# Attention in half-batch units of one pair of heads, and a first MLP that waits for half of batch 0

## The chip, the cores and the metric

The kernel runs on one core of a Trainium2 chip. The metric is the device time of one execution in microseconds (us), lower is better. TensorE (PE) multiplies and writes PSUM banks; VectorE (DVE), ScalarE (ACT) and GpSimd (POOL) work on what it leaves; the SP queue issues DMAs. Every engine runs its instructions in program order and waits on semaphores, so an instruction that waits also holds all that stand behind it on its engine.

## The reference, cut to what matters

Three stages follow each other. `q`, `k`, `v` are 4 batches x 8 heads x 576 positions x 64.

```python
q_d, k_d, v_d = means over groups of 4 positions      # 144 rows
out_up    = repeat(softmax_attention(q_d, k_d, v_d), 4)
out_local = softmax_attention(q, k, v, mask=|i - j| < 4)
x = (out_up + out_local) -> 2304 tokens x 512
h = x @ w_in;  g = s * relu(h)**2 + b;  y = g @ w_out           # d_ff 2048
out = ((y @ w_a) * (y @ w_b)) @ w2                              # d_ff 1536
```

Both MLPs are computed in float32 precision from pairs of a high and a low part ("hi" and "lo"), three matmuls for each product.

## The kernel before, in words

**Attention** goes by pairs of heads over a whole batch: 16 pairs (n), each 576 positions wide. A pair goes through three softmaxes, called jobs: POOLED (144 x 144, both halves together), LOCAL0 (windows 0 to 2 of 96 queries, 102 keys each) and LOCAL1 (windows 3 to 5). The steps of a job: PE turns q and k (`turn`, L467), ACT copies them out (L701, L703), DVE sums groups of four (L868), PE makes scores (L478, L493), DVE adds the mask and takes maxima (L875, L888, L890), POOL subtracts (L1073), ACT takes exponentials (L713, L719), DVE sums and inverts (L896 to L900), POOL normalises (L1081), PE turns the weights (L512, L517), ACT copies them (L726), PE multiplies with v (L538, L546), DVE adds pooled and local (L907, L917), and the result is split into hi on ACT (L776) and lo on DVE (L976).

**Boot.** The four pairs of batch 0 run alone, through 30 ticks, pair p six ticks behind pair p-1, in two sets of buffers ("kits") used in turn. In between, six of the sixteen weight blocks of the first MLP are split (hi on ACT L771, lo on DVE L971 or POOL L1088). The first `up_matmuls` stands at tick 28.

**First MLP.** 8 chunks of 288 tokens, 16 blocks each: 128 slots. In slot s PE does `attention(n, 2s)`, `up_matmuls(s)` (12 matmuls, L617, into the one bank HB), `attention(n, 2s+1)`, `down_matmuls(s-2)` (12 matmuls, L632). So an odd tick lies behind the up matmuls of its slot and an even tick in front of them. ACT does the even tick, `take_relu(s)` (L792), the odd tick, `split_g_hi(s)` (L797). DVE does the even tick, `square(s)` (L992, which needs the relu of this slot), the odd tick, `split_g_lo(s)` (L996). A pair has 8 slots, that is 16 ticks; the twelve pairs of batches 1 to 3 fill slots 0 to 95, and slots 96 to 127 have no attention. The order is written out by hand in `attention(n, at)` of each engine. At the third slot of a chunk ACT and DVE copy out the finished chunk (`take_acc`).

**Second MLP.** 6 chunks of 384 tokens, 12 blocks each: 72 steps of 24 matmuls up (L667) and 9 down (L681), with DVE L1051 and L1054, ACT L854 and L857 between. Its 12 weight blocks are split by ACT (L782) and DVE (L981): six within the last chunk of the first MLP, three right behind its last slot, three in front of the first steps.

## Time and profile before

| | us |
|---|---|
| median of 3 runs | 1070.12 (1069.66 to 1070.23) |
| the profiled execution | 1069.81 |
| span of its instructions | 1068.0 |
| up to the first matmul of the first MLP | 74.1 |
| start of its last up matmuls | 589.5 |

| engine | busy us | share of span |
|---|---|---|
| PE (matmul) | 1009.2 | 94% |
| DVE | 442.6 | 41% |
| ACT | 356.3 | 33% |
| POOL | 159.4 | 15% |

The share of PE is an average: in the first 74.1 us PE is busy for 46.4 us at a mean granted clock of 0.72, afterwards it is almost always busy.

### The profile page before, as it was taken

Reading aid. Unit: us, or ns where it says so; the run is one execution under the profiler, and the core shown is the slowest. Engines: PE = TensorE matmul, PEld = TensorE weight load, DVE = VectorE, ACT = ScalarE, POOL = GpSimd, SP = SyncE. Lnnn points to the kernel's source line nnn. Section 1 sums busy time; section 2 is a strip of 40 time slices with the busy share of each in tenths; the row PEclk is TensorE's granted clock in tenths of the full one; section 3 lists DMA queues with packets and bytes.
Section 4 is the critical chain, followed back from the end, with each engine's and each line's share of the span. In section 5 each row is a group of like instructions: output and inputs, shape, how many; then the busy total and the mean of one; then the engine's idle time right before and its main releaser. Section 6 shows DMA issues by size and latency. Waiting matters only on the chain.

```text
span 1068.0 us, 17004 instructions
## 1 busy us (share of the span) xinstructions
PE 1009.2 (94%) x6984; PEld 944.7 (88%) x6984; DVE 442.6 (41%) x800; ACT 356.3 (33%) x791; POOL 159.4 (15%) x126
## 2 busy tenths in 40 slices
PE   5678899999999999999999799999999999999997
PEld 4557889999999999999999699899899898998996
DVE  4768665565555655554345521211211212112111
ACT  3445444444344443344245421211211212212211
POOL 4545343122331223310000000000000000000000
PEclk9659999999999999999999899999999999999999
DMA  7343401121011210201033600010100100100000
GB/s 193 77 124 112 126 20 50 45 68 46 17 52 46 68 46 15 55 13 43 10 111 119 200 1 1 20 40 1 57 3 1 60 1 1 60 1 1 30 2 30
DMA packets 98829, 52.50 MB, mean 49 GB/s; under 512 B 60384, under 2 KB 92768, under 8 KB 98752
## 3 DMA queue, kind: packets, MB, share of 16 engines
q1 hardware_dynamic: 98608, 51.35, 17.3%
q8 instruction: 55, 0.90, 0.4%
q14 instruction: 22, 0.18, 0.1%
q10 hardware_dynamic: 144, 0.07, 0.0%
HBM read 41.97 MB, written 9.44 MB: 48 GB/s over the span
## 4 chain that ended last, share of the span: by engine, by line
PE 85%; DVE 6%; ACT 3%; POOL 3%; issue 2%; DMA 1%; SPq 0%; ACTq 0%; DVEq 0%; POOLq 0%
PE bank L667 28%; PE bank L632 18%; PE bank L617 17%; PE bank L681 13%; PE bank L546 2%; PE bank L493 2%; PE bank L517 2%; PE bank L467 1%; DVE relu L992 1%; POOL sm L1073 1%; PE bank L478 1%; POOL sm L1081 1%; PE bank L538 1%; POOL wx L1088 1%; PE bank L512 1%
## 5 line engine op out<-in xcount | busy, mean ns | idle before, releaser
L667 PE MATMUL bank<-x_hi,wx 128*128 128x384 f32 x1152 | 307.0, 337 | 11.8 <-DVE prod L1051 7.8
L632 PE MATMUL bank<-g_hi,wx 128*128 128x288 f32 x1024 | 234.2, 305 | 1.4 <-DVE o_sb L1004 1.4
L617 PE MATMUL bank<-wx 128*128 128x288 f32 x1536 | 230.7, 299 | 0.4 <-ACT relu L792 0.4
L667 PEld LDWEIGHTS bank<-x_hi,wx 128*128 128x128 f32 x1152 | 210.2, 188 | 17.3 <-issue 14.4
L617 PEld LDWEIGHTS bank<-wx 128*128 128x128 f32 x1536 | 211.8, 190 | 3.4 <-issue 2.8
L667 PE MATMUL bank<-x_lo,wx 128*128 128x384 f32 x576 | 193.5, 336 | 0.0
L632 PEld LDWEIGHTS bank<-g_hi,wx 128*128 128x128 f32 x1024 | 171.9, 189 | 9.5 <-issue 4.2
L1051 DVE TENSOR_TENSOR prod<-bank,a_sb 128x384 f32<-128x384 f32 x72 | 40.1, 558 | 314.5 <-ACT a_sb L854 314.5
L632 PE MATMUL bank<-g_lo,wx 128*128 128x288 f32 x512 | 151.5, 296 | 0.0
L992 DVE SCALAR_TENSOR_TENSOR relu<-relu,s_col 128x288 f32<-128x288 f32 x128 | 81.7, 638 | 166.4 <-ACT relu L792 166.2
L854 ACT ACTIVATE a_sb<-bank 128x384 f32<-128x384 f32 x72 | 35.3, 491 | 303.7 <-PE bank L667 303.7
L681 PE MATMUL bank<-wx,p_hi 128*128 128x512 f32 x432 | 134.4, 392 | 0.0
L667 PEld LDWEIGHTS bank<-x_lo,wx 128*128 128x128 f32 x576 | 108.6, 188 | 2.8
L792 ACT ACTIVATE relu<-bank 128x288 f32<-128x288 f32 x128 | 52.6, 411 | 173.7 <-PE bank L617 173.7
L632 PEld LDWEIGHTS bank<-g_lo,wx 128*128 128x128 f32 x512 | 96.7, 189 | 0.0
L797 ACT ACTIVATE g_hi<-relu,b_col 128x288 fp32r<-128x288 f32 x128 | 68.5, 535 | 80.4 <-DVE relu L992 80.4
L1081 POOL TENSOR_TENSOR sm<-sm,stat 96x612 f32<-96x612 f32 (+1 forms) x46 | 56.3, 1224 | 246.5 <-DVE stat L900 246.5
L681 PEld LDWEIGHTS bank<-wx,p_hi 128*128 128x128 f32 x432 | 80.1, 188 | 13.4
L996 DVE SCALAR_TENSOR_TENSOR g_lo<-relu,b_col,g_hi 128x288 fp32r<-128x288 f32 x128 | 70.6, 552 | 41.7 <-ACT g_hi L797 41.7
L681 PE MATMUL bank<-wx,p_lo 128*128 128x512 f32 x216 | 85.5, 396 | 0.0
L1054 DVE TENSOR_TENSOR p_lo<-prod,p_hi 128x384 fp32r<-128x384 f32 x72 | 40.2, 559 | 42.6 <-ACT p_hi L857 42.6
L857 ACT ACTIVATE p_hi<-prod 128x384 fp32r<-128x384 f32 x72 | 37.8, 526 | 46.2 <-DVE prod L1051 46.2
(67 smaller groups left out, 821.4 us busy)
## 6 DMA issues: line engine op xcount, KB each, us to landing
nat<-in_q SPq DMA_DIRECT2D x32, 144.0 KB, 2.9
nat<-in_k SPq DMA_DIRECT2D x32, 144.0 KB, 3.2
vnat<-in_v SPq DMA_DIRECT2D x32, 144.0 KB
o_transposed<-o_sb SPq DMA_DIRECT2D x8, 576.0 KB, 3.2
o_raw<-o_transposed SPq DMA_DIRECT2D x6, 768.0 KB, 4.7
out<-y SPq DMA_DIRECT2D x18, 256.0 KB, 2.2
vwin<-in_v SPq DMA_DIRECT2D x32, 120.0 KB
raw<-in_moe_w_a SPq DMA_DIRECT2D x12, 256.0 KB, 3.1
```

The source lines that it names most:

```text
L617: mm = nc.tensor.matmul(HB[:, 0:HALF], wi(w, kd, f), xs(x, c % 2)[:, kd], start=(kd == 0 and j == 0), stop=(kd == KD - 1 and j == 2))
L632: mm = nc.tensor.matmul(ACC[o][:, 0:HALF], wo(w, f, o), g[:, slot % GB, :], start=(f == 0 and j == 0), stop=(f == F1 - 1 and j == 2))
L667: mm = nc.tensor.matmul(dst[:, 0:CH2], wab(w, f, j * KD + kd), x[:, kd, :], start=(kd == 0 and m == 0), stop=(kd == KD - 1 and m == 2))
L681: mm = nc.tensor.matmul(ACC[tt], x[:, f % GB, tt * P:(tt + 1) * P], rows2(w, f), start=(f == 0 and m == 0), stop=(f == F2 - 1 and m == 2))
L792: nc.scalar.activation(relu[:, slot % 2, :], HB[:, 0:HALF], ACT.Relu).then_inc(r_ready, 1)
L797: nc.scalar.activation(g_hi[:, slot % GB, :], relu[:, slot % 2, :], ACT.Identity, bias=b_col[:, 0:1])\
L857: nc.scalar.activation(p_hi[:, f % GB, :], prod[:, f % 2, :], ACT.Copy).then_inc(ph_ready, 1)
L992: nc.vector.scalar_tensor_tensor(r, r, s_col[:, 0:1], r, ALU.mult, ALU.mult).then_inc(q_ready, 1)
L996: nc.vector.scalar_tensor_tensor(g_lo[:, slot % GB, :], relu[:, slot % 2, :], b_col[:, 0:1], g_hi[:, slot % GB, :].bitcast(f32), ALU.add, ...
L1051: nc.vector.tensor_tensor(prod[:, f % 2, :], bank[:, 1, 0:CH2], a_sb[:, f % 2, :], ALU.mult)\
L1054: nc.vector.tensor_tensor(p_lo[:, f % GB, :], prod[:, f % 2, :], p_hi[:, f % GB, :].bitcast(f32), ALU.subtract).then_inc(pl_ready, 1)
L1081: nc.gpsimd.tensor_tensor(x, x, d, ALU.mult).then_inc(p_ready, 1)
```

## The change

Attention goes by units u of one pair of heads over **half** a batch (288 queries): 32 units in the order batch, half, pair. The first unit of a batch and pair ("leads(u)") turns k for the whole batch and sums v; kT, pooled k and pooled v are kept for the second half. The three jobs of a pair become one pooled softmax of 72 x 144 for each head and one local one of three windows in each unit. There are four kits in the boot; only four units (batch 0, first half) run there, four ticks apart, and unit 4 begins five ticks ahead of slot 0. A unit then has 8 ticks, that is 4 slots, but runs through 12 ticks, so that neighbours overlap. Units 4 to 31 fill slots 0 to 111. The 1e-9 of the denominator becomes a 103rd column of the local scores, so the local sum needs no add. Four blocks of weights are split in the boot, the others in slots 0 to 11. Of the second MLP's blocks six are split in the last chunk and six behind the work of its first six steps.

```diff
+PER_UNIT = 2 * F1 // PAIRS
+LEAD = 5
+BOOT_SKEW = 4
+BOOT_TICKS = 23
+BOOT_BLOCK_TICKS = (-16, -12, -8, -4)
+EARLY2 = 6
...
+        def start(u):
+            return BOOT_SKEW * u - BOOT_TICKS if alone(u) else PER_UNIT * (u - PAIRS) - LEAD
+        def at_tick(g, t):
+            return [u for u in range(NU) if start(u) + t == g]
```

PE:

```diff
+            def turn_k(u):
...
+                    pe.wait_ge(ptl_taken, bank_before(u))
+            def scores(u):
...
+                pe.wait_ge(qp_ready, u + 1)
...
+                pooled_scores(0).then_inc(sp_half, 1)
+                for w in range(GW):
+                    for e in (1, 0):
+                        mm = local_scores(e, w)
+                mm.then_inc(sl_ready, 1)
+                pe.wait_ge(sp_half, u + 1)
+                pooled_scores(1).then_inc(sp_ready, 1)
+            def turn_pooled(u):
+                pe.wait_ge(pp_ready, u + 1)
...
+            def turn_local(u):
+                pe.wait_ge(pl_done, u + 1)
...
+            def attention(g):
+                for u in at_tick(g, 9):
+                    values(u)
+                for u in at_tick(g, 7):
+                    turn_local(u)
+                for u in at_tick(g, 5):
+                    turn_pooled(u)
+                for u in at_tick(g, 3):
+                    scores(u)
+                for u in at_tick(g, 0):
+                    if leads(u):
+                        turn_k(u)
+                for u in at_tick(g, 1):
+                    turn_q(u)
...
+            for g in range(-BOOT_TICKS, 0):
+                attention(g)
             for slot in range(SLOTS):
...
+                attention(2 * slot)
+                up_matmuls(*divmod(slot, F1))
+                attention(2 * slot + 1)
```

ACT, its `attention(g)`:

```diff
+                for u in at_tick(g, 11):
+                    split_x_hi(u)
+                for u in at_tick(g, 10):
+                    take_up(u)
+                for u in at_tick(g, 8):
+                    take_local(u)
+                for u in at_tick(g, 6):
+                    take_pooled(u)
+                for u in at_tick(g, 0):
+                    if leads(u):
+                        take_k(u)
+                for u in at_tick(g, 1):
+                    take_q(u)
+                for u in at_tick(g, 4):
+                    exp_pooled(u)
+                for u in at_tick(g, 5):
+                    exp_local(u)
```

DVE, where `maxima(u)` adds the mask, takes the local maxima, then the pooled maxima and their shift:

```diff
+            def weigh_local(u):
+                dve.wait_ge(el_ready, u + 1)
+                nc.vector.tensor_reduce(denl(u), kits[kit(u)]["sml"][:], X, ALU.add).then_inc(sum_ready, 1)
+                dve.wait_ge(sum_ready, u + 1)
+                nc.vector.reciprocal(denl(u), denl(u)).then_inc(recl_ready, 1)
...
+            def attention(g):
+                for u in at_tick(g, 11):
+                    split_x_lo(u)
+                for u in at_tick(g, 10):
+                    take_values(u)
+                for u in at_tick(g, 6):
+                    weigh_local(u)
+                for u in at_tick(g, 4):
+                    weigh_pooled(u)
+                for u in at_tick(g, 1):
+                    if leads(u):
+                        sum_k(u)
+                for u in at_tick(g, 2):
+                    sum_q(u)
+                for u in at_tick(g, 3):
+                    maxima(u)
```

POOL:

```diff
+            def attention(g):
+                for u in at_tick(g, 7):
+                    normalise_local(u)
+                for u in at_tick(g, 4):
+                    subtract(u)
+                for u in at_tick(g, 5):
+                    normalise_pooled(u)
+                for u in at_tick(g, 6):
+                    if leads(u):
+                        sum_v(u)
...
+            for slot in range(SLOTS):
+                c, f = divmod(slot, F1)
+                attention(2 * slot)
+                attention(2 * slot + 1)
+                if c == 0 and f + BOOT_BLOCKS < F1 and f % 2 == 1:
+                    split_w_lo(f + BOOT_BLOCKS)
```

The bodies of the steps do what their names said before, on half the queries.

## Rows read from the trace of the kernel before

**Rows 1.** Timeline of PE: first turn, first matmuls of slots 0, 48, 56, 116, 127.
```profile
6.82 2.15 PE L467 MATMUL bank<-ident,nat 96*128 96x96 f32 x12 [6.82 <-DMA nat<-in_k]
...
74.10 3.25 PE L617 MATMUL bank<-wx 128*128 128x288 f32 x12
...
289.93 1.84 PE L617 MATMUL bank<-wx 128*128 128x288 f32 x12
...
323.26 1.83 PE L617 MATMUL bank<-wx 128*128 128x288 f32 x12
...
554.39 1.76 PE L617 MATMUL bank<-wx 128*128 128x288 f32 x12
...
589.46 1.75 PE L617 MATMUL bank<-wx 128*128 128x288 f32 x12
```

**Rows 2.** Windows: stretch, length; busy us and count by engine; PE clock, DMA share, GB/s.
```profile
0.00:74.10 74.10, 46.41 (x367) 37.23 (x367) 48.95 (x84) 31.89 (x76) 37.36 (x36) 0.72 0.55 136
...
74.10:156.10 82.00, 70.05 (x581) 64.50 (x580) 54.72 (x82) 39.65 (x84) 38.54 (x23) 0.96 0.31 86
```

**Rows 3.** Waits of PE from 156 to 590 us (the whole answer).
```profile
PE bank L632 <- DVE o_sb L1004: 1.4, 4, 0.5
```

**Rows 4.** Timeline of slot 52 and behind it: what follows the end of up matmuls.
```profile
307.88 0.77 PE L493 MATMUL bank<-kT,qT 64*96 64x102 f32 x12
307.98 0.41 ACT L792 ACTIVATE relu<-bank 128x288 f32<-128x288 f32 x1 [2.60 <-PE bank L617]
308.43 0.52 DVE L992 SCALAR_TENSOR_TENSOR relu<-relu,s_col 128x288 f32<-128x288 f32 x1 [1.20 <-ACT relu L792]
308.86 0.78 DVE L888 TENSOR_TENSOR sm<-bank,mask 96x612 f32<-96x612 f32 x1
```

**Rows 5.** Timeline of slots 51 and 52: a local sum, its inversion, and the normalisation; subtraction beside g_lo.
```profile
305.85 0.78 DVE L896 TENSOR_REDUCE stat<-sm 96x6 f32<-96x612 f32 x1
306.66 0.17 DVE L898 TENSOR_SCALAR stat<-stat 96x6 f32<-96x6 f32 x1
306.86 0.19 DVE L900 RECIPROCAL stat<-stat 96x6 f32<-96x6 f32 x1
...
307.12 1.21 POOL L1081 TENSOR_TENSOR sm<-sm,stat 96x612 f32<-96x612 f32 x1 [3.54 <-DVE stat L900]
...
310.39 0.50 DVE L996 SCALAR_TENSOR_TENSOR g_lo<-relu,b_col,g_hi 128x288 fp32r<-128x288 f32 x1
310.55 1.41 POOL L1073 TENSOR_TENSOR sm<-sm,stat 96x612 f32<-96x612 f32 x1 [2.21 <-DVE stat L890]
```

**Rows 6.** Timeline: the pooled shift on DVE, and the first exponentials behind it on ACT.
```profile
296.94 0.17 DVE L877 TENSOR_SCALAR stat<-stat 72x4 f32<-72x4 f32 x1
...
297.20 0.38 ACT L713 ACTIVATE sm<-bank,stat 72x144 f32<-72x144 f32 x1 [0.39 <-DVE stat L877]
...
297.57 0.36 ACT L713 ACTIVATE sm<-bank,stat 72x144 f32<-72x144 f32 x1
```

**Rows 7.** Groups by shape, whole run: busy us, mean ns; idle time before and its releaser.
```profile
L875 DVE TENSOR_REDUCE stat<-bank 72x4 f32<-72x576 f32 x16 | 12.0, 749 | 6.1 <-PE bank L478 6.1
...
L726 ACT ACTIVATE pts<-bank 102x576 f32<-102x576 f32 x32 | 20.7, 647 | 32.2 <-PE bank L517 32.0
...
L1066 POOL TENSOR_TENSOR vd<-vnat 72x256 f32<-72x256 f32 x16 | 12.8, 797 | 1.3
...
L1088 POOL TENSOR_TENSOR wx<-stage,wx 128x1024 fp32r<-128x1024 f32 x6 | 14.4, 2399 | 7.9 <-ACT wx L771 7.9
```

**Rows 8.** Timeline of PE in the boot: local scores of one job.
```profile
59.96 1.34 PE L493 MATMUL bank<-kT,qT 64*96 64x102 f32 x12
```

**Rows 9.** Timeline of PE: first matmul of the second MLP's second step.
```profile
606.97 0.66 PE L667 MATMUL bank<-x_hi,wx 128*128 128x384 f32 x1 [6.56 <-DVE prod L1051]
```

**Rows 10.** Windows in the ramp, columns as in rows 2.
```profile
122.00:124.00 2.00, 0.19 (x4) 0.19 (x6) 2.00 (x3) 0.35 (x1) 0.00 (x0) 1.00 0.00 0
...
126.00:128.00 2.00, 2.00 (x10) 2.00 (x10) 0.00 (x0) 1.17 (x7) 0.00 (x0) 0.50 1.10 255
```

More of the change, by code:

```diff
@@ L306, in pt_bank, with place, leads, pair @@
-        def pt_bank(n):
-            return 4 * kit(n) + 2 if alone(n) else 1
-        def o_bank(n, kind):
-            return 4 * kit(n) + (1 if kind == LOCAL0 else 0) if alone(n) else 0
-        def boot_tick(at, tick_of):
-            return [p for p in range(PAIRS) if at - BOOT_SKEW * p == tick_of]
+        def place(u):
+            return u // (2 * PAIRS), u // PAIRS % 2, u % PAIRS
+        def leads(u):
+            return place(u)[1] == 0
+        def pair(u):
+            i, _, p = place(u)
+            return PAIRS * i + p
@@ L457, in _ @@
         def _(pe):
-            def turn(n, t):
-                if t == 0:
-                    pe.wait_ge(nat_in[kit(n)], 64 * uses(n))
-                    past(pe, o_taken, job(before(n), LOCAL1))
-                    past(pe, pt_taken, job(before(n), LOCAL1))
-                if t == 3 and not alone(n):
-                    pe.wait_ge(turn_taken, 4 * n + 1)
-                for u in range(GW):
-                    mm = nc.tensor.transpose(bank[:, turn_bank(n, t), u * WQ:(u + 1) * WQ],
-                                             nat(n)[:, t // 2, GW * (t % 2) + u, :], ident[0:WQ, 0:WQ])
-                mm.then_inc(turn_ready, 1)
@@ L705, in exps @@
-            def exps(n, kind):
-                if kind == POOLED:
-                    past(act, pt_ready, job(before(n), LOCAL1))
-                    act.wait_ge(shift_ready, n + 1)
-                    at = s_bank(n, POOLED)
-                    for e in range(2):
-                        for half in range(2):
-                            j = 2 * e + half
-                            done = nc.scalar.activation(sm_pooled(n)[:, e, half], bank[0:GH, at + e, half * G:(half + 1) * G],
-                                                        ACT.Exp, bias=shift(n)[:, j:j + 1], scale=1.0 / POOL ** 2,
-                                                        accum_out=den(n, POOLED)[:, j:j + 1])
-                    done.then_inc(exp_ready, 1)
-                else:
-                    act.wait_ge(sub_ready, local(n, kind))
-                    nc.scalar.activation(sm_flat(n, kind), sm_flat(n, kind), ACT.Exp).then_inc(exp_ready, 1)
@@ new lines, in take_q, with exp_pooled @@
+            def take_q(u):
+                act.wait_ge(q_turned, u + 1)
+                past(act, sl_ready, before(u))
+                nc.scalar.activation(kits[kit(u)]["qT"][:], bank[:, turn_q_bank(u), 0:HALF], ACT.Copy, scale=SC)\
+                  .then_inc(q_taken, 1)
+            def exp_pooled(u):
+                act.wait_ge(shift_ready, u + 1)
+                past(act, ptp_ready, before(u))
+                for e in range(2):
+                    done = nc.scalar.activation(kits[kit(u)]["smp"][:, e], bank[0:GH, base(u) + 2, e * G:(e + 1) * G],
+                                                ACT.Exp, bias=shift(u)[:, e:e + 1], scale=1.0 / POOL ** 2,
+                                                accum_out=denp(u)[:, e:e + 1])
+                done.then_inc(ep_ready, 1)
@@ new lines, in take_local, with take_up @@
+            def take_local(u):
+                act.wait_ge(ptl_ready, u + 1)
+                past(act, o_ready, before(u))
+                nc.scalar.activation(kits[kit(u)]["ptl"][:], bank[0:WK, base(u):base(u) + 2, 0:HALF], ACT.Copy)\
+                  .then_inc(ptl_taken, 1)
+            def take_up(u):
+                act.wait_ge(o_ready, u + 1)
+                past(act, o_taken, before(u))
+                nc.scalar.activation(kits[kit(u)]["up"][:], bank[:, base(u) + 2, HALF:HALF + GH], ACT.Copy,
+                                     scale=1.0 / POOL).then_inc(up_taken, 1)
@@ L833, in _ @@
                         split_w2_hi(f // 2 - 2)
-            for f in range(6, 9):
-                split_w2_hi(f)
             take_acc(NCH - 1)
@@ L1124 @@
+            for g in range(-BOOT_TICKS, 0):
+                attention(g)
+                if g in BOOT_BLOCK_TICKS and BOOT_BLOCK_TICKS.index(g) % 2 == 1:
+                    split_w_lo(BOOT_BLOCK_TICKS.index(g))
+            for slot in range(SLOTS):
+                c, f = divmod(slot, F1)
+                attention(2 * slot)
+                attention(2 * slot + 1)
+                if c == 0 and f + BOOT_BLOCKS < F1 and f % 2 == 1:
+                    split_w_lo(f + BOOT_BLOCKS)
 _INS = ['q', 'k', 'v', 'moe_w_in', 'moe_w_out', 'moe_s', 'moe_b', 'moe2_w_a', 'moe2_w_b', 'moe2_w_out']
```

908 lines of the change are left out of this document (347 added, 561 removed).

## The prediction

> **What bounds the kernel now.** I read the timeline of PE first. The first MLP starts at 74.1 us, and the first matmuls of its last slot at 589.46 [rows 1]. Slots without attention follow each other every (589.46 - 554.39) / 11 = 3.19 us; eight slots with one pair in them take 323.26 - 289.93 = 33.33 us, so a pair costs PE 33.33 - 25.5 = 7.8 us. The waits of PE show that from 156 to 590 us it waits for 1.4 us in all, and only for a chunk to be copied out [rows 3]: there PE is the bound, and every wait put into its queue lengthens the run. The windows show two stretches where it isn't [rows 2]. In the boot PE is busy for 46.4 of 74.1 us at a mean granted clock of 0.72, DVE for 49.0: a chain of short steps in order over four engines. From 74.1 to 156.1, the ramp, 16 slots take 82.0 us where 66.7 would do: 15.3 lost, while weight blocks are split on busy engines. The third loss is where the second MLP begins [rows 9].
>
> **The time.** Terms are summed against the profiled execution, 1069.8 us, which is 0.3 below the median; I keep one decimal less than that.
>
> **1. Boot.** Before, four whole pairs; after, four half units, 23 ticks in place of 28 up to the first up matmuls. Durations are from the chains and groups [rows 4 to 8]. I walk one unit from the end of its scores to the end of the next unit's, in the program order of the four ticks that they share. Pooled branch: mask 0.8, local maximum 0.8, pooled maximum 0.45 (estimate: half the elements of L875), shift 0.2, two exponentials 0.8 behind it [rows 6], add and inversion 0.4, start of POOL 0.3, normalisation 0.8 (L1066 as the nearest, 256 elements for 288): 4.5 with the hand-overs. Then, in PE's order, turn_pooled 0.5 and turn_q 0.6; take_q stands ahead of exp_local on ACT, so 0.45, then 0.7 for the exponential; take_up 0.3; take_values 0.45 ahead of weigh_local on DVE, 1.0; normalisation 1.5 with its start; turn_local 1.1 and scores 1.85 (PE at the slower clock: twelve passes take 1.34 [rows 8] against 0.77 at the faster [rows 4]). Sum 12.9 us. The first scores end at about 10.8 (first turn at 6.8 [rows 1], k now first in the queue), the fourth at 10.8 + 12 + 2 x 13 = 48.8. Behind it values(3) ends 10.9 later, scores(4) 1.85, and PE then has turn_pooled(4) in front of the first up matmuls, 4.5 + 0.5: 66.6. At the faster clock it would be 60. I take **64**, bounds 57 and 72. Gain 10 us. The loads don't bound it: 3.3 MB up to the fourth unit's k and q, and more than 40 us for them.
>
> **2. PE work in the slots.** Before, 12 pairs in slots: 12 x 7.8 = 94. After, 28 units at half a pair. The passes per pair are the same, but for pooled values (twice as many matmuls of half the width), against fewer changes between attention and MLP matmuls: 3.9 us each, bounds 3.6 and 4.2. 28 x 3.9 = 109. **+15 us.** This work came out of the boot, where it was hidden in a chain.
>
> **3. New waits of PE.** A unit has 12 ticks, and most of its steps are one tick from the step that feeds them. One tick is the 12 matmuls of an up or a down, 12 x 0.133 = 1.59 us. So I set each chain against what PE does meanwhile.
> a) turn_local, tick 7, at g = 2 mod 8: in front of the up matmuls of a unit's second slot. Its feeder weigh_local, tick 6, is an odd tick, so on DVE behind square(s), which waits for the relu of up(s). From the end of up(s): relu starts 0.10 later, square 0.45 later, the next on DVE 0.43 later [rows 4], the sum's successor 0.81 later, POOL 0.26 behind the inversion's start, and 1.21 to normalise [rows 5], 0.06 to PE: 3.3. PE has only down(s-2), 1.59. Wait 1.75, x 28 = **49 us**. Behind it in PE's queue stand the up matmuls, and with them relu, square and all of the slot.
> b) turn_pooled, tick 5, behind scores, tick 3, with one up and one down between (3.5 us with pooled score 1 and the change of kind). The pooled branch takes 4.5 (term 1). Wait 1.0, x 28 = **28 us**. Moving the pooled maximum behind the local one costs 1.6 of it.
> c) scores, tick 3, needs sum_q of DVE, which stands behind square and take_values: 0.10 + 0.45 + 0.43 + 0.4 + 0.45 + 0.05 = 1.9 against 1.59. Wait 0.3, x 28 = **8 us**.
> d) turn_k, tick 0, odd, is directly behind the up matmuls and needs take_local, which ACT does behind the relu of the same slot: 0.10 + 0.41 + 0.65 (L726 [rows 7]) and a hand-over, less 0.1 by which two copies overlap, 1.1, with nothing on PE to cover it. Only the 12 leading units in slots have it: **13 us**.
> Sum 98 us. Bounds: 60 (a alone at 1.75 and a chunk of d) and 115 (each 0.2 us later). The same walk through the code before gives feeders two ticks ahead of p_turn for each job, and the trace shows no wait there [rows 3]; that is my reason to trust it.
> In a and b POOL works while DVE runs an instruction with two SBUF inputs. In the trace a POOL pass beside g_lo takes 1.41, one alone 1.21 [rows 5]. The Trainium skill says in "GPSIMD Engine Reference", Key points, that GpSimd shares its SBUF interfaces with VectorE and contends with such instructions; the trace agrees. By that rule each normalisation beside g_lo would be 0.2 longer, 6 us over 28 units, which the upper bound holds.
>
> **4. Ramp.** Slots 0 to 11 now split one block each. In slots 3, 7 and 11 POOL's split (2.4 us, L1088 [rows 7]) stands between subtract and normalise_pooled, and waits for ACT's split ahead of it: turn_pooled comes some 3.3 us later still, three times, 10 us. DVE's split in slots 2, 6 and 10 delays maxima by about 1: 3. With the copies of the chunks as before it is about the 15.3 that is lost now. **0 us**, bounds -8 and +12.
>
> **5. Start of the second MLP.** The second step starts at 606.97 behind 6.56 us of idle time [rows 9], since nine blocks are split ahead of the first product; its first matmul lasts 0.66, about twice a matmul at full clock, and one more block is split ahead of the next product. Six blocks early, and the rest behind the work of the steps: the next product no longer waits. Without it the third step would begin some 9.5 us earlier: 6.6, and an estimate of 3 for the slow matmuls and the second wait. **-9.5 us**, bounds -10 and 0 (if the loads, now begun only when the last unit has been split in slot 111, come late).
>
> Removed instructions of DVE and ACT (one add for each local sum, half the k work at the second half) lie beside PE's work: nothing. DMAs: k and v are loaded once per batch and pair as before, q and the windows in halves; SP only waits longer. Nothing, as long as each is issued a slot ahead.
>
> **Sum:** 1069.8 - 10 + 15 + 98 + 0 - 9.5 = 1163.3. I say **1163 us**.
>
> **The rivals.**
> A. *The waits are covered and the boot halves (faster).* The place is weigh_local to turn_local: it decides whether POOL is done within 1.59 us of the end of up(s). For it speaks only that DVE and POOL are idle much of the time; against it, that normalising alone takes 1.21 and stands behind four other steps. Without term 3 the sum is 1065; with a boot down to 41 us as well, 1042. Chance 0.08 for both; a hundredth or two of it ends within 0.2% of before.
> B. *The waits draw down PE's clock.* The ramp shows it: after 1.9 us of idle time in the stretch from 122 us, the granted clock is 0.50 from 126 to 128 [rows 10], which is the lower level, 1.2 GHz. Over the whole ramp it is 0.96 [rows 2], so most gaps did nothing. The low stretch of 2 us or more cost at least 1 us of PE's work; I take 1.7. If every unit has one: 28 x 1.7 = 48, so 1211. Chance 0.2. The Trainium skill, "TensorE: Matmul & The Clock Gate", section on HAM oscillation, warns of just this, gaps between bursts that bring back the half clock; it would make 1211 out of 1163, and this trace agrees in one gap of several.
> C. *Only the waits that hang on one whole chain come (a and d, and b in part):* about 65 of the 98 us, 1130. For it: estimates of half-size steps may be too long. Chance 0.24.
> D. *The boot isn't shorter,* as take_q stands behind turn_pooled on PE and ahead of exp_local on ACT, all of it cold: first up at 74 or later, the sum 1173 or more. Chance 0.08.
> My own sum (1145 to 1185) has 0.4.
>
> **How the numbers follow.** 0.2% (2 us) is what a measurement of this kernel can tell from no change. The range 1105 to 1215 takes in C with short steps, my sum with its bounds, D and B, and leaves out A and the tails. All but A are slower: slower 0.9, same 0.02, faster 0.08.
>
> **What would show it.** In the waits of PE: the turn of local weights on POOL's normalisation, 28 times at about 1.7 us; the turn of pooled weights on POOL at about 1.0; the turn of k on ACT's copy, 12 times 1.1; scores on DVE's sum of q at 0.3. In the timeline of PE: first up matmuls at 60 to 68 us; four slots taking 20 us in place of 16.7; slots 112 to 127 at 3.19. In the windows a clock of 1.0 behind the boot (B if under 0.95). At the start of the second MLP no gap over 2 us. I am wrong if four slots take 17 us or less, or if PE's waits in the slots sum to less than 50 us.

## The result, and the profile after

The changed kernel takes **1223.74 us** (median of 4 runs, 1223.55 to 1225.18) against 1070.17 for the kernel before beside it: the ratio is 1.144, 95% interval 1.142 to 1.146. Slower, as forecast, but by 154 us where 93 were forecast, and 9 us beyond the upper end of the range.

The page of the profile after, its parts 1, 2 and 4:

```profile
span 1223.1 us, 17523 instructions
...
PE 1043.7 (85%) x7112; PEld 971.9 (79%) x7112; DVE 447.3 (37%) x834; ACT 359.6 (29%) x823; POOL 157.3 (13%) x144
...
PE   4466688878788788787787899999999999999998
...
PEclk9998888899988999988899999999999999999999
...
PE 68%; DVE 13%; POOL 7%; issue 6%; ACT 4%; DMA 1%; POOLq 0%; SPq 0%; DVEq 0%
```

DVE is busy 5 us longer than before, ACT 3, POOL 2 less and PE 34 longer, most of it in matmuls at the lower clock (in e4 below, where fewer are slow, PE is busy for 1010.9 us). What is new is that PE stands still in the slots, six to eight tenths busy from 61 to about 700 us, and that the chain that ended last runs for 24% of the span through DVE, POOL and ACT. The waits of PE from 70.5 to 752 us (first up at 70.7, last up at 751.3); before, it waited for 1.4 us from 156 us on [rows 3] and for 11.8 in the ramp. Columns: sum in us, times, longest:

```profile
PE bank L522 <- POOL smp L983: 61.3, 28, 6.2
PE bank L530 <- POOL sml L989: 51.2, 28, 3.4
PE bank L472 <- issue: 13.0, 12, 1.1
PE bank L497 <- DVE pooledq L818: 6.5, 27, 0.3
```

In the order of these rows: turn_pooled, turn_local, turn_k, scores. They are the four waits of the prediction's term 3, with the counts 28, 28, 12 and about 28. One of the first row, 5.25 us, ends at 70.26, ahead of the first up matmuls, and so belongs to the boot. Without it turn_pooled waits 56.0 us in 27 units, and the four sum to 127 us: 1.57 in each unit behind the ramp and three times 6.1 in it for turn_pooled, 1.85 and in the first unit 3.4 for turn_local. "issue" at turn_k means that the record names no releaser; what follows below shows that it is take_local.

The timeline of one unit, with its two waits on POOL:

```profile
218.31 1.85 PE L582 MATMUL bank<-wx 128*128 128x288 f32 x12
218.37 0.79 DVE L827 TENSOR_TENSOR sml<-bank,mask 96x612 f32<-96x612 f32 x1 [0.30 <-PE bank L503]
219.19 0.79 DVE L829 TENSOR_REDUCE stat<-sml 96x6 f32<-96x612 f32 x1
219.90 0.44 DVE L832 TENSOR_REDUCE stat<-bank 72x2 f32<-72x288 f32 x1
220.06 1.21 POOL L977 TENSOR_TENSOR sml<-sml,stat 96x612 f32<-96x612 f32 x1 [14.61 <-DVE stat L829]
...
220.38 0.91 DVE L834 TENSOR_SCALAR stat<-stat 72x2 f32<-72x2 f32 x1
...
221.32 0.38 ACT L667 ACTIVATE smp<-bank,stat 72x144 f32<-72x144 f32 x1 [0.70 <-DVE stat L834]
...
222.62 0.66 POOL L983 TENSOR_TENSOR smp<-smp,stat 72x288 f32<-72x288 f32 x1 [1.36 <-DVE stat L840]
...
223.34 0.45 PE L522 MATMUL bank<-ident,smp 72*72 72x72 f32 x4 [1.57 <-POOL smp L983]
```

The chain is mask, two maxima, shift, exponentials, inversion, POOL, PE. The shift (L834) takes 0.91 us on 72 x 2 numbers, against 0.17 before on 72 x 4 [rows 6]: it runs beside POOL's subtraction, which began 0.32 earlier. It does so in every unit (count, then shortest, median and longest in ns):

```profile
L834 DVE TENSOR_SCALAR stat<-stat x32: 905/909/911, 13.4 to 683.3; 72x2 f32<-72x2 f32 x32
```

The windows of a stretch around 182 us (columns as in rows 2), and PE's timeline there:

```profile
178.00:180.00 2.00, 1.16 (x9) 0.92 (x7) 1.80 (x4) 0.84 (x3) 0.43 (x1) 1.00 0.46 139
180.00:182.00 2.00, 1.00 (x10) 1.00 (x11) 0.00 (x0) 0.00 (x0) 0.95 (x1) 1.00 0.38 86
182.00:184.00 2.00, 2.00 (x10) 1.86 (x9) 0.00 (x0) 0.00 (x0) 0.00 (x0) 0.52 0.00 0
184.00:186.00 2.00, 0.91 (x6) 0.73 (x6) 0.52 (x1) 0.95 (x2) 0.00 (x0) 0.50 0.00 0
186.00:188.00 2.00, 2.00 (x11) 2.00 (x10) 0.37 (x1) 1.07 (x2) 0.00 (x0) 0.50 0.00 0
188.00:190.00 2.00, 2.00 (x26) 1.80 (x25) 1.53 (x4) 0.00 (x0) 0.00 (x0) 0.77 0.00 0
```

```profile
181.00 0.70 PE L530 MATMUL bank<-ident,sml 96*102 96x96 f32 x6 [1.84 <-POOL sml L989]
181.49 2.72 PE L582 MATMUL bank<-wx 128*128 128x288 f32 x12
185.30 1.19 PE L472 MATMUL bank<-ident,natk 96*128 96x96 f32 x6 [1.09 <-issue]
```

PE idles 1.84 us in front of turn_local. In the windows from 182 to 188 the granted clock is 0.50 to 0.52, the lower level (1.2 GHz). The twelve up matmuls behind the turn take 2.72 in place of 1.85, turn_k 1.19 in place of 0.69, and the down matmuls run slowly too: this slot lasts 8.84 us where one with a turn of k and without the fall needs 6.3. Such a stretch at the lower clock is called a fall here. From the starts of the up matmuls, 15 of the 28 units have such a slot, with 1.25 to 2.55 us too much each, 26.6 in all: 10 of the 12 in which k is turned, and 5 of the other 16. In all 15 the lower level begins 0.2 to 1.5 us behind the start of turn_local (here 1.1), so it follows the gaps of turn_pooled and turn_local and comes before that of turn_k. The ramp has three more falls (the clock is 0.50 from 98 to 103, from 125 to 130 and from 149 to 157 us); they aren't among the 15. Slots 112 to 127, without attention, come every 3.19 us as before.

**The ledger**, in spans, that is from the first to the last instruction of the profiled execution (1223.1 - 1068.0 = 155.1). Up to the first up matmuls: 70.7 - 74.1 = -3.4. From the first up to the last: (751.3 - 70.7) - (589.5 - 74.1) = +165.2. Behind it: 471.8 - 478.5 = -6.7.

From first up to last up, 128 slots at 3.19 us are 408 in both. Before, 12 pairs at 7.8 add 94, and 13 are left, as much as PE's waits there (11.8 and 1.4). After, 28 units at 3.48 and 12 times 0.53 for turning k (both read from e11 below) add 104, the waits 127, the clock 27, and 15 are left. So +165 is +114 waits, +27 clock, +10 work and +15 that no run takes apart. Two things that go into the 15 can be seen: a wait costs more than the idle time of its row (in e2 a unit becomes 2.05 us shorter when its wait of 1.85 goes), and the ramp has its own falls.

### The profile page after: what moved, and what is told of

The parts are those of the page before. It is cut to its first block, busy times and chain, and to the rows that moved or that the text cites. A ratio compares the mean times of both kernels' runs of the same rounds, so it can differ in the third digit from the quotient of the medians.

```text
span 1223.1 us, 17523 instructions
## 1 busy us (share of the span) xinstructions
PE 1043.7 (85%) x7112; PEld 971.9 (79%) x7112; DVE 447.3 (37%) x834; ACT 359.6 (29%) x823; POOL 157.3 (13%) x144
## 4 chain that ended last, share of the span: by engine, by line
PE 68%; DVE 13%; POOL 7%; issue 6%; ACT 4%; DMA 1%; POOLq 0%; SPq 0%; DVEq 0%
PE bank L624 25%; PE bank L582 15%; PE bank L638 11%; PE bank L594 7%; POOL sml L989 3%; PE bank L530 2%; DVE sml L827 2%; DVE stat L829 2%; ACT relu L739 2%; POOL smp L983 2%; DVE stat L845 2%; DVE stat L834 2%; DVE relu L901 1%; PE bank L503 1%; PE bank L497 1%
## 5 line engine op out<-in xcount | busy, mean ns | idle before, releaser
L582 PE MATMUL bank<-wx 128*128 128x288 f32 x1536 | 259.2, 323 | 0.0
L582 PEld LDWEIGHTS bank<-wx 128*128 128x128 f32 x1536 | 231.7, 208 | 4.4 <-issue 4.3
L594 PEld LDWEIGHTS bank<-g_hi,wx 128*128 128x128 f32 x1024 | 179.6, 197 | 0.7 <-issue 0.5
L901 DVE SCALAR_TENSOR_TENSOR relu<-relu,s_col 128x288 f32<-128x288 f32 x128 | 66.0, 515 | 296.0 <-ACT relu L739 296.0
L594 PE MATMUL bank<-g_lo,wx 128*128 128x288 f32 x512 | 155.6, 304 | 0.0
L594 PEld LDWEIGHTS bank<-g_lo,wx 128*128 128x128 f32 x512 | 100.8, 197 | 0.0
L905 DVE SCALAR_TENSOR_TENSOR g_lo<-relu,b_col,g_hi 128x288 fp32r<-128x288 f32 x128 | 76.2, 596 | 47.5 <-ACT g_hi L744 45.7
L638 PEld LDWEIGHTS bank<-wx,p_hi 128*128 128x128 f32 x432 | 80.1, 188 | 13.4
L977 POOL TENSOR_TENSOR sml<-sml,stat 96x612 f32<-96x612 f32 x32 | 38.6, 1206 | 365.9 <-DVE stat L829 365.9
L530 PE MATMUL bank<-ident,sml 96*102 96x96 f32 x192 | 26.6, 284 | 64.9 <-POOL sml L989 64.9
L522 PE MATMUL bank<-ident,smp 72*72 72x72 f32 x128 | 16.2, 257 | 73.0 <-POOL smp L983 73.0
```

The costliest lines, as they stand in the source:

```text
L530: mm = nc.tensor.transpose(bank[0:WK, base(u) + e, w * WQ:(w + 1) * WQ], kits[kit(u)]["sml"][:, GW * e + w, 0:WK], ident[0:WQ, 0:WQ])
L582: mm = nc.tensor.matmul(HB[:, 0:HALF], wi(w, kd, f), xs(x, c % 2)[:, kd], start=(kd == 0 and j == 0), stop=(kd == KD - 1 and j == 2))
L594: mm = nc.tensor.matmul(ACC[o][:, 0:HALF], wo(w, f, o), g[:, slot % GB, :], start=(f == 0 and j == 0), stop=(f == F1 - 1 and j == 2))
L638: mm = nc.tensor.matmul(ACC[tt], x[:, f % GB, tt * P:(tt + 1) * P], rows2(w, f), start=(f == 0 and m == 0), stop=(f == F2 - 1 and m == 2))
L901: nc.vector.scalar_tensor_tensor(r, r, s_col[:, 0:1], r, ALU.mult, ALU.mult).then_inc(q_ready, 1)
L905: nc.vector.scalar_tensor_tensor(g_lo[:, slot % GB, :], relu[:, slot % 2, :], b_col[:, 0:1], g_hi[:, slot % GB, :].bitcast(f32), ALU.add, ...
```

## The experiments

Unless another kernel is named, each edit is made to the changed kernel. "Before" ran beside each of them at 1068.9 to 1070.1 us. A time without an interval is one profiled execution, good for differences of more than a few us.

**e1: fill the gaps.** Small matmuls into unused columns of a bank stand ahead of the two waits on POOL, so that PE doesn't idle.

```diff
+            def fill(u, tick, count):
+                if alone(u):
+                    return
+                pe.wait_ge(r_ready, (start(u) + tick) // 2)
+                for _ in range(count):
+                    nc.tensor.matmul(HB[:, 384:512], ident[:, :], ident[:, :], start=True, stop=True)
             def turn_pooled(u):
+                fill(u, 5, 7)
...
             def turn_local(u):
+                fill(u, 7, 9)
```

> The changed kernel with 9 small matmuls of the identity (128 columns, into the unused columns of bank HB) ahead of the wait for the normalised local weights, and 7 ahead of the wait for the pooled ones, in units 4 to 31; the waits themselves stay. They need 1.1 to 1.4 us, less than the 1.85 and 1.57 us that TensorE stands idle there. Theory (the idle gaps draw the clock down, and it is the clock that makes some units 22 to 24.5 us long where the others take 20.1): all units take 20.1 to 20.5 us, the granted clock is at 1.0 from slot 12 on, and the run takes 1165 to 1185 us. Rival 1 (the clock falls for something else than idle time, or the filling costs as much as it saves): still some 13 long units, 1215 to 1235 us. Rival 2 (the long units are not the clock's work): clock at 1.0, but the units are as long as before.

Measured: 1196.69 us, 27.0 less, with all the waits of the dependencies in place. The windows from 130 to 500 us, first of the changed kernel, then of e1:

```profile
130.00:500.00 370.00, 298.29 (x2442) 277.57 (x2441) 165.13 (x328) 122.17 (x314) 75.62 (x67) 0.93 0.13 35
```

```profile
130.00:500.00 370.00, 351.39 (x3102) 334.78 (x3102) 171.61 (x344) 127.53 (x329) 77.55 (x69) 0.99 0.15 37
```

The clock rises from 0.93 to 0.99, and from 160 to 700 us it is 1.00. Two units without k still take 40.3 us, so the fill replaces idle time and adds none; what goes is the excess of the 15 slots. Their falls cost 27 us, as counted from the slots. The run is 12 us above the range that I expected, since slots of 6.3 us that I had counted as falls are the ordinary ones in which k is turned. Two more things stand in this trace. turn_k isn't filled and still waits 1.09 us twelve times, and no slot behind the ramp has a fall: that gap alone brings none. And the three falls of the ramp are still there. The other 127 us are not the work of these 15 falls.

**e2: turn_local alone.** DVE sums the local exponentials a tick earlier, on the even tick, ahead of the square.

```diff
-                for u in at_tick(g, 6):
+                for u in at_tick(g, 5):
                     weigh_local(u)
```

> The changed kernel with weigh_local on VectorE at tick 5 in place of 6, that is in front of the square of its slot and not behind it. Theory (the wait of 1.85 us comes from the order relu, square, sum, inversion, normalisation against one down on TensorE): the wait of turn_local on GpSimd goes from 65 us to under 10, a unit without a clock fall takes 18.3 us in place of 20.1, and with fewer falls the run takes 1130 to 1172 us. Rival (the normalisation is late for a cause further up, the exponential or GpSimd itself): the wait stays above 1 us a unit, 1195 us or more.

Measured: 1135.59 us, 88 less. The waits of PE, whole run:

```profile
PE bank L522 <- POOL smp L983: 73.0, 32, 6.2
PE bank L472 <- issue: 13.0, 12, 1.1
PE bank L530 <- POOL sml L989: 12.8, 4, 3.4
```

Two units take 36.2 in place of 40.3, so a unit is 2.05 shorter: the wait of 1.85 in each unit is gone, the four left are in the boot, and the wait of turn_pooled is untouched. 28 x 2.05 = 57; the clock is 1.00 from 145 us on, so the 27 of e1 are in it too. The gaps of turn_pooled (1.57) and turn_k (1.09) are all still there, and behind the ramp not one fall follows them. One line moved by one tick is worth more than half of what the change cost.

**e3: turn_pooled alone.** PE turns the pooled weights a tick later, behind the up matmuls.

```diff
-                for u in at_tick(g, 5):
+                for u in at_tick(g, 6):
                     turn_pooled(u)
```

> The changed kernel with turn_pooled on TensorE at tick 6 in place of 5, behind the up matmuls of its slot. Theory (the pooled branch is about 1.6 us longer than the up and down that cover it): the wait of turn_pooled goes from 73 us to under 15, the unit takes 18.6 us, the wait of turn_local stays at 1.85, and the run takes 1140 to 1185 us. Rival (the wait moves on to turn_local, since the chain behind is bound by it): the wait of turn_local grows to 3 us or more a unit, 1215 us or more.

Measured: 1147.77 us, 76 less. turn_pooled waits 23.1 us in 7 units (73.0 in 32), turn_local 54.5 (64.9), first up 59.5 in place of 70.7. turn_local's wait is 1.37 in 12 units, which take 18.1, and 2.07 in the 12 leading ones behind the ramp. So the wait of 1.57 is real, and it can be undone alone; in the plain units the rival's move of the wait to turn_local didn't come. The clock is 0.95 from 130 to 500 us: behind the ramp four falls are left, each behind a gap of 2.07, and none behind one of 1.37. So neither of the two gaps alone does what both in one unit do: 1.57 alone, none of 24 (e2); 2.07 alone, four of 12 (e3); 1.57 and then 1.85, 15 of 24 (the changed kernel).

**e4: the three together.** e2, e3, and ACT copies the local weights a tick earlier, ahead of the relu, which is what turn_k needs.

```diff
-                for u in at_tick(g, 8):
+                for u in at_tick(g, 7):
                     take_local(u)
```

> The changed kernel with weigh_local at tick 5, turn_pooled at tick 6, and take_local on ScalarE at tick 7, in front of the relu of its slot, so that turn_k finds its bank free. Theory (waits of TensorE and the clock falls that they cause are the whole loss in the slots): waits of TensorE in the slots under 20 us in all, a unit takes 16.7 to 17.2 us, clock at 1.0 from slot 12 on, 1080 to 1105 us. Rival (the smaller units cost TensorE more work than half a pair each): waits gone but 18 us a unit, 1120 us or more.

Measured: 1102.01 us, ratio 1.030 (1.029 to 1.032). The wait of turn_k is gone from the list (13.0 before), so "issue" was ACT's copy. turn_local still waits 36.1 us in 29 units: 2.5 in each of the four of the boot, about 1.44 in the 12 leading ones, where POOL's sum of v stands ahead of the local normalisation, and 0.61 in the others. The misordered ticks, with the falls that came with them, cost 122 us of the 154, and still the new scheme doesn't pay.

**e5: the kernel before, with the new start of the second MLP only.** Six blocks split in the last chunk, the others behind the first steps, one in each.

```diff
+EARLY2 = 6
...
-            for f in range(6, 9):
-                split_w2_hi(f)
...
-                    if c == 0 and 9 + f < F2:
-                        split_w2_hi(9 + f)
...
+                    if c == 0 and EARLY2 + f < F2:
+                        split_w2_hi(EARLY2 + f)
```

> The kernel before, with nothing of the change but the order of the second MLP's weight blocks: six split in the last chunk of the first MLP, the other six behind the work of the second MLP's first six steps, and their loads issued in that order. Theory (this part alone is a gain, since the second step no longer waits for blocks 6 to 10): the idle time of 6.6 us in front of the second step goes, no fall of the clock there, 1060 to 1064 us. Rival (the loads or the copy-out then bind the second step): a wait of some 3 us or more stays, 1067 us or more.

Measured: 1064.11 us, ratio 0.995 (0.994 to 0.997): 5 us faster. The wait of PE at the first steps, before and in e5:

```profile
PE bank L667 <- DVE prod L1051: 7.8, 2, 6.6
```

```profile
PE bank L669 <- DVE prod L1047: 2.5, 2, 1.3
```

Behind the last up matmuls e5 is 6.6 us shorter (471.9 for 478.5). 5.3 are in this row: both first steps still wait 1.26 for the product. The other 1.3 are the slow matmuls: before, the clock is 0.50 from 603 to 608 us, and the second step takes 5.7 us from 606.97 in place of the 4.35 of the first; in e5 the clock is 1.00 there. The run as a whole gains less, as its first slots take 1.6 us longer.

**e6: pooled maxima ahead of the mask.** To take the stretched shift out of the chain of turn_pooled.

```diff
             def maxima(u):
                 h, at = place(u)[1], base(u)
+                dve.wait_ge(sp_ready, u + 1)
...
+                nc.vector.tensor_reduce(mxp(u), src, X, ALU.max).then_inc(mxp_ready, 1)
+                dve.wait_ge(mxp_ready, u + 1)
+                nc.vector.tensor_scalar(shift(u), mxp(u), -1.0 / POOL ** 2, None, ALU.mult).then_inc(shift_ready, 1)
                 dve.wait_ge(sl_ready, u + 1)
...
                 nc.vector.tensor_reduce(mxl(u), kits[kit(u)]["sml"][:, :, 0:WK], X, ALU.max).then_inc(mxl_ready, 1)
-                dve.wait_ge(sp_ready, u + 1)
...
-                nc.vector.tensor_scalar(shift(u), mxp(u), -1.0 / POOL ** 2, None, ALU.mult).then_inc(shift_ready, 1)
```

> The changed kernel with the pooled maxima and their shift ahead of the mask and the local maxima on VectorE. Theory (the small shift instruction lasts 0.9 us in place of 0.2 since it meets GpSimd's subtraction, and that is why the pooled weights come 1.57 us late where 1.0 was forecast): the shift lasts under 0.25 us, the wait of turn_pooled is 0.8 to 1.1 us in most units, the run takes 1195 to 1212 us. Rival (the shift is slow of itself, as its statistics come straight from a reduction): it lasts 0.9 as before, the wait is above 1.4.

Measured: 1219.41 us, nearly nothing, and above the range that I expected. turn_pooled still waits 1.50. The timeline of e6:

```profile
257.59 0.17 DVE L826 TENSOR_SCALAR stat<-stat 72x2 f32<-72x2 f32 x1
...
259.34 1.54 DVE L901 SCALAR_TENSOR_TENSOR relu<-relu,s_col 128x288 f32<-128x288 f32 x1
259.36 1.21 POOL L977 TENSOR_TENSOR sml<-sml,stat 96x612 f32<-96x612 f32 x1 [13.53 <-DVE stat L834]
```

The shift is back to 0.17, in all 32 units. The instruction that now runs beside POOL's subtraction is the square, and it takes 1.54 in place of 0.50; behind it stand the sums of the pooled shares. So the shift is not slow of itself. The price of running beside POOL's subtraction went to the DVE instruction that stood there now, and so stayed in the chain.

**e7: the ramp.** POOL's splits of blocks 7, 11 and 15 two slots later, away from turn_pooled's normalisation.

```diff
-                if c == 0 and f + BOOT_BLOCKS < F1 and f % 2 == 1:
-                    split_w_lo(f + BOOT_BLOCKS)
+                if c == 0 and f % 4 == 1:
+                    for block in (f + 2, f + 4):
+                        if block > BOOT_BLOCKS and block < F1:
+                            split_w_lo(block)
```

> The changed kernel with GpSimd's splits of blocks 7, 11 and 15 two slots later, behind normalise_local of the next unit, so that none stands between subtract and normalise_pooled. Theory (slots 3, 7 and 11 take 10 us in place of 5.3 for this order): those three intervals go to 5.3 to 6 us, the run takes 1203 to 1214 us. Rival (ScalarE's split or the loads hold them): they stay at 9 or more, 1220 us or more.

Measured: 1210.69 us, 13 less. The slots 3, 7 and 11 take 6.6 in place of 10.0 us (5.27 later on): 3.4 three times, the 3.3 of term 4, and 10 of the 13 us.

**e8: the boot.** turn_q ahead of turn_pooled in PE's order.

```diff
-                for u in at_tick(g, 5):
-                    turn_pooled(u)
...
                 for u in at_tick(g, 1):
                     turn_q(u)
+                for u in at_tick(g, 5):
+                    turn_pooled(u)
```

> The changed kernel with turn_q ahead of turn_pooled in TensorE's order of a tick, which matters in the boot alone: take_q then stands no longer behind the whole pooled branch, and exp_local stands behind take_q. Theory (that is what makes a boot unit 13 us): 10 us for each of the first three units, the first up matmuls at 60 to 64 us in place of 70.7, the run at 1213 to 1218 us. Rival (the boot unit is bound elsewhere, by VectorE's order): 12.5 us or more a unit, 69 us or later, 1222 or more.

Measured: 1209.83 us. First up at 64.9 in place of 70.7, a boot unit 11.2 in place of 13.1 us. It gives 6 of the 14 us; the other 8 are in the falls: 13 slots have one, with 18.7 us too much, in place of 15 with 26.6, though the slots are in the same order. So how many fall varies between kernels whose slots are alike, and a difference of under ten us between two such kernels says little on the part that was changed.

**e9: five orders.** e4, e6, e7 and e8 together, and POOL's sum of v a tick later, behind both normalisations.

```diff
-                for u in at_tick(g, 6):
+                for u in at_tick(g, 7):
                     if leads(u):
                         sum_v(u)
```

> The changed kernel with weigh_local at tick 5, turn_pooled at tick 6 and take_local at tick 7 as before, and besides the pooled maxima first, turn_q ahead of turn_pooled in TensorE's order, GpSimd's splits of blocks 7, 11 and 15 two slots later, and sum_v behind normalise_local. Theory (what is left in the slots is order too): first up matmuls at 50 to 54 us, the three long intervals of the ramp gone, a unit 16.6 to 17.3 us, waits for GpSimd under 30 us in all, 1062 to 1080 us. Rival (the contention between GpSimd's subtraction and whichever VectorE instruction stands beside it keeps the local chain as long as it is): the wait of turn_local stays at 36 us, 1085 us or more.

Measured: 1103.83 us, ratio 1.033 (1.030 to 1.035), no better than e4. turn_local waits 22.6 (36.1 in e4), turn_pooled 13.4 (23.9), the ramp's first twelve slots take 59.5 us in place of 81.7, first up at 56.0. The sum missed its range (1062 to 1080). But there is a new wait, and with it falls of the clock in its slots:

```profile
PE bank L547 <- DMA vwin<-in_v: 17.1, 9, 2.3
```

**e10: the local branch earlier.** e9 with exp_local (ACT) at tick 4 and weigh_local (DVE) at tick 4, behind weigh_pooled.

```diff
-                for u in at_tick(g, 5):
+                for u in at_tick(g, 4):
                     exp_local(u)
...
-                for u in at_tick(g, 5):
-                    weigh_local(u)
                 for u in at_tick(g, 4):
                     weigh_pooled(u)
+                for u in at_tick(g, 4):
+                    weigh_local(u)
```

> As e9_five_orders, and besides exp_local at tick 4, ahead of split_g_hi of its slot on ScalarE, and weigh_local at tick 4, ahead of split_g_lo on VectorE. Theory (the local chain then meets no instruction of the MLP before the normalisation): the wait of turn_local under 8 us in all, first up matmuls at 45 to 50 us, since a boot unit takes 9.5 to 10 us in place of 11.2, a unit in the slots 16.2 to 16.8 us, 1045 to 1060 us, which is faster than the kernel before. Rival (g_hi and g_lo late by 1 to 2 us now hold down_matmuls or the next relu): new waits of TensorE on g_lo or relu, and no gain over e9.

Measured: 1092.3 us, ratio 1.020 (1.018 to 1.023), where 1045 to 1060 were expected. turn_local waits 6.4 us in all, two units without k take 32.97 us, as one pair of heads before (33.33 [rows 1]). Two that turn k take 41.4, and 18.4 us of waiting for `vwin` are left. The SP queue of e10 shows why (an issue, its length, the tile):

```profile
275.49 0.83 SPq L319 DMA_DIRECT2D natq<-in_q  x2
276.36 1.01 SPq L326 DMA_DIRECT2D natk<-in_k  x2
289.09 0.74 SPq L334 DMA_DIRECT2D vnat<-in_v  x2
289.88 0.76 SPq L347 DMA_DIRECT2D vwin<-in_v  x2
```

v (L334) waits 11.7 us, until POOL's sum of the pair before ends at 289.07, and the windows of the next unit stand behind it in the queue. The values of that unit waited for them (1.83 us at 293.41).

**e11: the windows ahead of k and v.** e10 with this one edit on SP.

```diff
                             load_q(u + 1)
-                            if leads(u + 1):
-                                load_k(u + 1)
-                                load_v(u + 1)
                     for u in at_tick(g, 10):
                         if u >= PAIRS and u + 1 < NU:
                             load_vwin(u + 1)
+                    for u in at_tick(g, 2):
+                        if u >= PAIRS and u + 1 < NU and leads(u + 1):
+                            load_k(u + 1)
+                            load_v(u + 1)
```

> The kernel of e10 with one thing moved: SP loads the value windows of a unit (L347 to L353) ahead of the k and v of the next pair, whose v waits for POOL's sum of the pair before. In e10 the windows of nine units were issued late (289.9 us in one case, 13.5 us after the q issued in the same slot at 275.5, behind v issued at 289.1) and PE waited 18.4 us in all for them, with clock falls behind. Theory 1 (the wait of L547 is a matter of SP's order alone): the wait goes, the pairs of leading units become about 35 to 37 us instead of 41.4, time 1055 to 1078 us. Theory 2 (what the leading units lose lies in the transfers themselves or in the next thing that is late, v for POOL's sum): the wait of L547 goes, but a wait of about the same size stands at another line of the leading units, time 1085 to 1095 us.

Measured: **1059.96 us**, ratio **0.991 (0.989 to 0.993)**: faster than the kernel before by 10 us, or 1%. The windows from 130 to 500 us, and the waits of PE in the whole run:

```profile
130.00:500.00 370.00, 364.68 (x3282) 345.35 (x3281) 241.97 (x443) 161.20 (x419) 99.08 (x90) 1.00 0.18 47
```

```profile
PE bank L523 <- POOL smp L984: 12.8, 7, 3.8
PE bank L498 <- DVE pooledq L819: 12.0, 28, 2.0
PE bank L531 <- POOL sml L990: 6.6, 7, 1.8
PE bank L473 <- DMA natk<-in_k: 5.0, 1, 5.0
```

No wait for `vwin` is left. Two units that turn k take 34.0 us, the others 33.0, at a full clock, and nowhere behind the ramp does a slot show a fall. PE is the bound again; of the four waits only the 0.24 us of scores are left behind the ramp.

In spans, e11 is 17.8 us shorter up to the first up matmuls (56.3 for 74.1), 15.7 longer from there to the last (531.1 for 515.4), and 6.7 shorter behind it. So two thirds of the gain are the new start of the second MLP, which e5 has without the new attention. What the smaller boot saves the slots take back, 10 us of it as work of PE, as term 2 said they would.

**e12: the sum of v early.** e11 with sum_v back at tick 6.

> As e11, with POOL's sum of v (L967, L970: 1.49 + 0.83 us) put back a tick earlier, ahead of both normalisations, as in the kernel after. Theory 1: in the leading units POOL is 2.3 us later with the normalised shares, so turn_pooled and turn_local wait in each of them: 5 to 25 us slower than e11. Theory 2 (SP's wait for the sum is what delays the leading units): v and what follows it are issued earlier and the time is the same as e11 or up to 10 us shorter.

Measured: 1079.79 us, ratio 1.010 (1.008 to 1.012), 20 us slower than e11. turn_local waits 25.0 us in 17 units in place of 6.6 in 7. POOL's timeline in e12 has the sum between the two normalisations:

```profile
281.29 0.66 POOL L984 TENSOR_TENSOR smp<-smp,stat 72x288 f32<-72x288 f32 x1 [0.67 <-DVE stat L841]
281.92 1.28 POOL L968 TENSOR_TENSOR vnat<-vnat 72x512 f32<-72x512 f32 x1
283.27 0.84 POOL L971 TENSOR_TENSOR vd<-vnat 72x256 f32<-72x256 f32 x1
284.07 1.20 POOL L990 TENSOR_TENSOR sml<-sml,stat 96x612 f32<-96x612 f32 x1
```

## Why the prediction was right in its cause and too low in its size

**The steps that failed.** The forecast was 60 us too low, and two steps of it hold most of that. The sum took nothing for the clock, which cost 27 us in the slots. And term 3b took 0.2 us for the pooled shift, which took 0.91, and turn_pooled waited 1.57 us a unit where 1.0 was forecast, 16 us in all. The rest are the boot (7) and the ramp (6), each too low, the start of the second MLP (3), and some 5 us by which waits cost more than the idle time that the walk gave them; against these, PE's work came out 5 us below the forecast.

**The waits (term 3)** are the mechanism. e2 and e3 take the two large ones out alone, and e4 takes out that of turn_k with them.
- a) turn_local, 1.75 forecast: 1.84 to 1.86 in the 24 units behind the ramp, +3 us.
- b) turn_pooled, 1.0 forecast: 1.57, 16 us too low. What failed is the duration of the pooled shift. I took 0.2 from a row where POOL was idle beside it [rows 6]; here it takes 0.91. I had named POOL's contention as 0.2 us for each normalisation beside g_lo, from the one pair in rows 5. That much came: in the slots POOL's local normalisation takes 1.38 us for 1.21, behind a g_lo that began earlier. What I missed is that DVE can pay as well, and more. The Trainium skill, "GPSIMD Engine Reference", Key points, says that the SBUF interfaces are shared with VectorE, with contention for DVE instructions in a 2-port performance mode or with two SBUF inputs. The runs agree for g_lo and for the square of e6 (1.54 for 0.50), which read two tensors; the shift reads one, and no run shows in which mode it ran. It is not shown either that the shift alone made the wait: e6 takes it out of the chain, another instruction pays, and the wait falls by 0.07.
- c) scores, 0.3 forecast: 0.24.
- d) turn_k, 1.1 x 12 forecast: 1.09 x 12.

**The clock (rival B, which I priced at 48 us with a chance of 0.2).** It came, but in 15 units of 28: 26.6 us from the slots, 27.0 by e1. My own case held none of it, and this is the largest part of the miss. The row I had pointed at it [rows 10]: a gap of 1.9 us and the low level behind it, and I had just forecast 28 gaps of 1.75. Of the four gaps of 1.4 us and more that PE has in the ramp before (1.40, 1.75, 1.75, 1.91), one has a fall behind it. From that I could have put a share of the gaps into the sum, an estimate of 28/4 x 1.7 = 12 us; I took it for all or nothing. The Trainium skill, "TensorE: Matmul & The Clock Gate", tells of two ways to such falls: in "HAM oscillation" the waits between the bursts are longer than the gaps here, and under "A second HAM failure mode", right behind it, PE idles only briefly between groups of matmuls. The trace is nearer to the second, with the number beside it: 15 falls behind 24 pairs of gaps of 1.57 and 1.85 us.

**Boot (term 1), 64 forecast, 70.7 measured.** The walk was right for a unit: 13.1 against 12.9, and the fourth scores end at 50 against 48.8. Behind it the last part took 20.7 where the walk says 17.8. And I had then set 64 between the walk's 66.6 and 60 for a faster clock, which never came: in the boot a pass of scores takes 372 ns, in the slots 245. Rival D (74 or later) did not come; e8 shows that its cause, the order of turn_q and turn_pooled, costs 6 us.

**PE's work (term 2), +15 forecast:** +10. In e11 a unit adds 3.72 us to its slots, of which 0.24 are the wait of scores, so 3.48, under the lower bound of 3.6; turning k adds 0.53.

**Ramp (term 4), 0 forecast:** the mechanism of the three slots is right in size (3.4 each, e7), but the loss was not "about the 15.3 that is lost now". The first twelve slots take 81.7 us, 21 more than three undisturbed units of 20.14, with three falls among them.

**Start of the second MLP (term 5), -9.5 forecast:** -6.7, and -6.6 in e5. I said that no wait would be left; 1.26 us stand at each of the first two steps, so the waits gave 5.3. The 3 us for the slow matmuls and the second wait were an estimate; the slow matmuls gave 1.3.

**The sum again.** 1163, + 27 clock, + 16 and + 3 for b and a, - 2 for c, + 7 boot, + 6 ramp, - 5 work, + 3 start: 1218, against 1223.7 measured. The 5 or 6 that are left fit what e2 shows, that a wait of 1.85 costs 2.05 (24 times 0.2); that this is their cause was not tried. Rival A fell: nothing covers these waits. Rival C fell: the waits came whole. Rival B came in half of the units, and with it the time left the range.

**What stays open:** why a given pair of gaps brings a fall and the next, as long, doesn't. Shown is that the falls come behind turn_local, that filling the two gaps of turn_pooled and turn_local takes them away (e1), and that each of the two alone brings none or few (e2, e3). Falls are more frequent where k is turned (10 of 12 against 5 of 16), but in e1 and e2 turn_k's gap stays and none is there; in e8 the two groups are nearer, 7 of 12 and 6 of 16. How e11 stands without each of its other edits was tried for the sum of v only (e12).

## What to carry to other kernels

When work moves from a hidden place into slots that PE fills, walk every chain from the last matmul that feeds it to the first that needs it, and count the ticks by engine: here a step fed from an odd tick one tick earlier had 1.6 us of cover for 3.3 us of work, and one tick moved on one engine was worth 88 us, some 27 of them through the clock. Add to each gap a price for the clock, as a share of the gaps, as soon as one row shows a fall behind a gap of that size. And read the queue of SP in order: a load that waits for a free buffer holds the loads behind it, and that may only show once the engines are fast.

## What the runs showed of the hardware that I had not expected

- **A tiny VectorE instruction ends only with the GpSimd pass beside it.** The shift of 72 x 2 numbers takes 0.17 us alone (e6, all 32) and 0.91 (all 32) beside POOL's 1.21 us subtraction. It ends 0.02 behind POOL (220.38 + 0.91 against 220.06 + 1.21). The square, 0.50 alone, begins with POOL in e6, takes 1.54 and ends 0.31 behind it. That looks as if the instruction gets little done until POOL ends, rather than as if both ran at a lower rate; no run here isolates it. The pooled maximum, which reads PSUM and overlapped the subtraction by 0.28, kept its 0.44. GpSimd's own pass stays at 1.21 in both.
- **The column of the granted clock can read 1.00 where matmuls are slow.** In the boot after, it stands at 1.00, while this view of single matmuls (count, then median, mean and longest in ns) shows scores at the slow duration, and the same line in the slots:

```profile
L503 PE MATMUL bank<-kT,qT x60: 372/373/485, 9.6 to 64.6; 64*96 64x102 f32 x60
```

```profile
L503 PE MATMUL bank<-kT,qT x48: 245/247/326, 263.6 to 324.7; 64*96 64x102 f32 x48
```

  Two runs with the same boot differ in the column too: from 0 to 60 us it reads 0.77 before and 1.00 in e5, and scores have a median of 372 and 373 ns. For the boot the durations are the safer reading.
